# An attention and two-layer mixture kernel: one block's score and gate work reordered, and each expert's row numbers kept one expert earlier

## The reference, cut to what matters

```python
def _attn_ref(q, k, v):            # q, k, v: (2, 8, 576, 64)
    scores = scale * np.matmul(q, k.transpose(0, 1, 3, 2))
    kth = np.partition(scores, -top_k, axis=-1)[..., -top_k:-top_k + 1]     # top_k = 32
    scores = np.where(scores >= kth, scores, -1000000000.0)
    attn = np.exp(scores - np.max(scores, axis=-1, keepdims=True))
    attn = attn / (np.sum(attn, axis=-1, keepdims=True) + 1e-09)
    return np.matmul(attn, v)

def _moe_ref(x, w_in, w_out):      # x: (1152, 512), w_in: (512, 2048), w_out: (2048, 512)
    h = x @ w_in
    return (h * np.cos(h)) @ w_out

def _moe2_ref(x, w_gate, w1, w2, capacity):    # 8 experts, w1: (8, 512, 1024), w2: (8, 1024, 512)
    expert_idx = np.argmax(x @ w_gate, axis=1)
    # gate_w[i]: softmax weight of the chosen expert; each expert takes its first `capacity` rows
    h = np.maximum(np.einsum('ecd,edf->ecf', disp, w1), 0.0)
    y = np.einsum('ecf,efd->ecd', h, w2)
    out[i] = gate_w[i] * y[expert_idx[i], pos[i]]
```

## Time and profile before

| what | value |
|---|---|
| median of 3 runs | 662.5 us (661.8 to 662.95) |
| the profiled execution, its own time | 662.5 us |
| its span, first to last instruction | 660.8 us |
| TensorE matmul busy | 611.5 us, 93% |
| TensorE weight load busy | 548.3 us, 83% |
| VectorE busy | 526.6 us, 80% |
| ScalarE busy | 437.7 us, 66% |
| GpSimd busy | 289.7 us, 44% |
| chain that ended last | PE 66%, ACT 15%, POOL 8%, issue 7%, DVE 3% |

### The profile page before, as it was taken

One profiled execution on the slowest core, in us unless ns is written; L12 is line 12 of the kernel. 1 busy time (PEld: TensorE's weight loads), 2 busy tenths in 40 slices (PEclk: granted clock), 3 DMA queues, 4 the chain that ended last, 5 costly groups with the idle time before them and its releaser, 6 DMA issues.

```text
span 660.8 us, 13481 instructions
## 1 busy us (share of the span) xinstructions
PE 611.5 (93%) x4302; PEld 548.3 (83%) x4302; DVE 526.6 (80%) x1017; ACT 437.7 (66%) x727; POOL 289.7 (44%) x294
## 2 busy tenths in 40 slices
PE   4778798899999999999999999999898999999994
PEld 3556696798897898998988978989687999999994
DVE  5999999988989979989989985016539877789751
ACT  2567478679679679688596796736438665667630
POOL 0376559457477366566474675821500111011111
PEclk9988599999999999999999999999899999999998
DMA  5874700000000000000000000060398675675400
GB/s 180 354 325 172 270 5 5 26 5 5 25 5 5 25 6 5 25 9 1 28 4 16 0 0 18 1 235 5 144 348 303 231 269 199 248 248 221 147 18 16
DMA packets 17792, 68.62 MB, mean 104 GB/s; under 512 B 1998, under 2 KB 6606, under 8 KB 15056
## 3 DMA queue, kind: packets, MB, share of 16 engines
q1 hardware_dynamic: 16000, 63.27, 25.8%
q0 software_dynamic: 1744, 4.73, 2.0%
HBM read 54.33 MB, written 14.45 MB: 104 GB/s over the span
## 4 chain that ended last, share of the span: by engine, by line
PE 66%; ACT 15%; POOL 8%; issue 7%; DVE 3%; DMA 0%; POOLq 0%; ACTq 0%; SPq 0%; DVEq 0%
PE p_a L1281 8%; PE p_o L1243 6%; PE p_b L1281 5%; PE p_s L1205 5%; PE p_b L1303 4%; PE p_t L1222 3%; PE p_s L1498 3%; PE p_b L1305 3%; PE p_b L1304 3%; PE p_t L1498 3%; PE p_t L1475 3%; POOL arena L678 3%; PE p_s L1475 3%; ACT arena L843 2%; POOL w_out_lo L717 2%
## 5 line engine op out<-in xcount | busy, mean ns | idle before, releaser
L374 DVE MAX8 top<-arena 128x8 f32<-128x576 f32 x288 | 201.1, 745 | 7.4 <-ACT arena L843 7.3
L377 DVE MATCH_REPLACE8 arena<-top,arena 128x576 f32<-128x576 f32 x216 | 158.6, 741 | 0.0
L678 POOL TENSOR_TENSOR arena<-arena,pen 128x576 f32<-128x576 f32 x72 | 100.7, 1421 | 57.1 <-ACT pen L850 57.1
L1243 PEld LDWEIGHTS p_o<-arena,probsT 128*128 128x128 f32 (+1 forms) x720 | 85.7, 191 | 12.8 <-ACT probsT L870 6.8
L1243 PE MATMUL p_o<-arena,probsT 128*128 128x65 f32 (+1 forms) x720 | 90.9, 273 | 5.6 <-ACT probsT L870 3.8
L870 ACT COPY probsT<-p_t 128x384 f32<-128x384 f32 x108 | 51.3, 480 | 53.9 <-PE p_t L1222 53.8
L1222 PE MATMUL p_t<-ident,arena 128*128 128x128 f32 x324 | 55.7, 284 | 13.2 <-ACT arena L862 13.2
L1281 PE MATMUL p_a<-xT,wff 128*128 128x128 f32 x512 | 66.0, 283 | 0.0
L1281 PE MATMUL p_b<-xT,wff 128*128 128x128 f32 x512 | 64.3, 279 | 0.0
L1303 PE MATMUL p_b<-w_out_lo,g_hi 128*128 128x512 f32 x144 | 62.5, 434 | 1.9 <-ACT h_sb L889 1.6
L1281 PEld LDWEIGHTS p_a<-xT,wff 128*128 128x128 f32 x512 | 60.8, 195 | 2.8 <-issue 2.4
(11 more groups left out here) (186 smaller groups left out, 1309.4 us busy)
## 6 DMA issues: line engine op xcount, KB each, us to landing
arena<-in_w SPq DMA_DIRECT2D x8, 2048.0 KB, 9.0
wff<-in_w SPq DMA_DIRECT2D x8, 2048.0 KB, 9.1
slot_rows<-y_now SPq DMA_DIRECT2D x1, 4626.0 KB, 14.7
wff<-in_w_out SPq DMA_DIRECT2D x1, 4096.0 KB, 12.2
wff<-in_w_in SPq DMA_DIRECT2D x1, 4096.0 KB, 22.0
wff<-slot_rows SPq DMA_DIRECT2D x8, 385.5 KB, 3.7
arena<-in_vones SPq DMA_DIRECT2D x2, 1300.0 KB, 16.8
q_sb<-in_q SPq DMA_DIRECT2D x36, 64.0 KB, 1.9
```

The costliest lines, as they stand in the source:

```text
L374: nc.vector.max(best, src).then_inc(top_step, 1)
L377: nc.vector.match_replace(work[:, a, :], best, src, LOWEST).then_inc(top_step, 1)
L678: nc.gpsimd.tensor_tensor(s_sb[:, t, :], s_sb[:, t, :], pen[:, t % 2, :], ALU.subtract).then_inc(masked, 1)
L1243: last = mm(p_o[q, lo:lo + n], probsT[:, g % 2, P * c + q.start:P * c + q.stop], vones[b][:, p, at:at + n], start=(k == 0), stop=(k == PAI ...
```

## The change

Two things move; nothing is added or taken away.

In block 1, GpSimd makes the bias and the masks of pair 0 of block 2 ahead of the gate product of part 2, and ScalarE does the last score copy, the penalties and the exponentials of that pair ahead of the cosines of parts 2 and 3.

In the experts, VectorE's `keep` for expert E no longer stands inside expert E behind the scaling of expert E-1's rows. It stands inside expert E-1, behind `low_x(E)` and ahead of the rest of the weight splitting for expert E. With the indices of that place, its second wait is for the sending of expert E-2's rows, whose sending starts in the same expert E-1.

```diff
@@ VectorE, expert @@
                 else:
                     scale_rows(E - 1, 1 - j, turn - 1 + j, n)
-                    keep(E, j, turn, n)
                 sum_unit(E, 2, n)
...
                 if more:
                     low_x(E + 1, n)
+                    keep(E + 1, 1 - j, turn + j, n)
                     low_w1(E + 1, 1 - j, range(4) if begin else (2, 3))
                     low_w2(E + 1, 1 - j, 0)
                 sum_unit(E, 4, n)
@@ GpSimd, body, block 1 @@
                     fraction(i - 1, 3)
+                    bias(i + 1, 0)
+                    masks(i + 1, 0)
                     gated(i - 1, 2)
-                    bias(i + 1, 0)
                     gated(i - 1, 3)
-                    masks(i + 1, 0)
                     bias(i + 1, 1)
@@ ScalarE, second_body, block 1 @@
                 copy_pT(i, 10)
+                scores(i + 1, 3)
+                pens(i + 1, 0)
+                copy_pT(i, 11)
+                exps(i + 1, 0)
                 cosines(i - 1, 1)
-                scores(i + 1, 3)
-                copy_pT(i, 11)
-                pens(i + 1, 0)
+                copy_o(i, 1)
                 high_g(i - 1, 2)
-                copy_o(i, 1)
                 high_g(i - 1, 3)
-                exps(i + 1, 0)
                 pens(i + 1, 1)
```

## The result

| | before | changed |
|---|---|---|
| median | 662.7 us (4 runs, 661.8 to 664.5) | 687.1 us (4 runs, 684.8 to 689.6) |
| ratio | | 1.037, 95% interval 1.031 to 1.042 |
| profiled execution, own time | 662.5 us | 684.2 us |
| its span | 660.8 us | 682.4 us |

The change made the kernel 24 us slower. The four timed runs of the changed kernel fall into two pairs, at 684.9 and 689.5 us, with mean granted clocks of 0.970 and 0.973 in the one and 0.956 and 0.958 in the other; the profiled execution belongs with the faster pair.

What follows compares the result with a forecast made beforehand. The prediction took TensorE's pace to bound the experts and a wait for ScalarE to bound the end of block 1. It summed 662.5 + 3.1 - 0.1 + 15.7 = 681.2 us, range 671 to 691.

Steps and rivals of the forecast that it cites:

- The bound: Expert loop: TensorE sets the pace, busy 20.37 of 20.40 us; VectorE's 3.6 us to spare must cover `keep`'s cost.
- Block 1, exponentials: End of block 1: exponentials done at 113.2 and 114.65, TensorE's transposes at 115.1 without a wait, winning 2.4 us there.
- Block 1, what is late next: Cosines now behind exponentials: remainder at 119.4, w_out matmul at 119.5; the 2.4 us given back and 0.35 more.
- Blocks 2 and 3: Table load inside the loop: block 2's multiplication with v 2.1 us late, block 3 up to 1.0 more; 3.1 together.
- The drain of the table load: ScalarE in block 1's part: the skill page adds a 1.38 us drain per switch, making 5.9 us instead of 3.1.
- Five stalls, with expert 6 free for lack of a load: Experts 1 to 5: `keep` waits for a sending beside the w1 load; expert 0 has no wait, expert 6 no load.
- Size of a stall: Experts: last packet 4.2 us behind `low_x`, 0.3 until VectorE goes on, 0.15 of copies; weight splitting 4.4 us late.
- The alternative that I wrote down: Experts: if the rows' moving clears nothing, each stall is 5.4 us and costs 4.2, 21 us in all.
- Cover: Experts: the sum of unit 5 comes 1.24 us before `turn_back`'s second half needs it, hiding that much of each stall.
- The five stalls together: Five experts: 4.4 - 1.24 = 3.15 us for TensorE in each, 15.7 us.
- The copies, -0.1: `keep`'s two copies: 0.14 us won in each of experts 6 and 7, 0.14 lost in expert 0; sum -0.1 us.
- The clock: Rival: TensorE's clock falls behind six new pauses in experts and block 2, 688 us in all; chance 0.14.

Runs made afterwards that it cites:

- block 1 alone: Kernel before with only the block 1 reordering, `keep` at its old place: 665.3 us, ratio 1.004.
- the kernels with the later w1: SyncE starts the w1 load one unit of TensorE later, put on the kernel with only `keep` moved (662.3 us) and on the changed kernel (666.0 us).
- `keep` alone: Kernel before with only `keep` moved into the previous expert behind `low_x`, block 1 as before: 686.4 us, ratio 1.036.
- The changed kernel with the later w1: Changed kernel, with SyncE starting the w1 load of the expert after next one unit of TensorE later: 666.0 us, ratio 1.006.
- the late `keep`: Kernel before with `keep` moved one expert earlier, but to that expert's end, behind the last `low_w2`: 661.5 us, ratio 0.9987.
- the filled pauses: Kernel with only `keep` moved, plus three extra unread TensorE matmuls before `turn_back`'s first half in experts 1 to 6: 682.7 us, ratio 1.030.
- the later w1: Control: kernel before with only the w1 load started one unit of TensorE later, `keep` at its old place: 662.4 us, ratio 1.000.
- `keep` in between: Kernel before with `keep` moved one expert earlier, behind `low_w1` and the first `low_w2`, ahead of the sum of unit 4: 665.4 us, ratio 1.005.
- `keep` with the later w1: Kernel before with `keep` moved as in the changed kernel and the w1 load started one unit of TensorE later: 662.3 us, ratio 1.000.

## Why the prediction was right, and where it was off

- **The bound.** That the experts run at TensorE's pace and that VectorE's spare time decides: right. The stretch without a stall takes 20.43 us, the others 24 to 26.
- **Block 1, exponentials.** Forecast done at 113.2 and 114.65, transposes at 115.1 without a wait; measured 113.2 and 114.6, transposes at 114.61 without a wait. Right.
- **Block 1, what is late next.** The remainder was put at 119.4 and the w_out matmul at 119.5; it came at 119.78. Right in kind, 0.3 us low. The wait is 3.5 us and not the 2.9 that I named as its sign, because TensorE also got there 0.35 us earlier, at 116.26.
- **Blocks 2 and 3.** Load done and multiplication with v at 123.05, measured 123.08; the transposition of x at 125.4, measured 125.52; block 3 up to 1.0 more, measured 0.75. Sum forecast 3.1, measured 2.74 at the last block and 3.25 at the first expert, 2.9 us (1.7 to 4.0 by its interval) in the runs with this part alone. Right. In the profiled execution the clock was at half from 119.6 to 123.0 us; this cost nothing at the multiplication with v, since the copy that it needs came no sooner (block 1 alone, at full clock, waits 1.28 us for that copy). A kernel with the old block 1 also loses time here in some executions, 1.6 us as the last section shows, and the profiled one of before was not of them. That the single pair of traces gave so nearly the forecast is in part luck.
- **The drain of the table load.** The Trainium skill's 1.38 us (ScalarE: Activation LUTs, What ACT_TABLE_LOAD costs) would have made this part 5.9 us. The new loads took 1.28 us and the next instruction followed at once (121.19 and 122.48, 167.81 and 169.10); the trace does not bear the drain out.
- **Five stalls, with expert 6 free for lack of a load.** Right, and shown by the kernels with the later w1: the w1 load beside the sending is the cause.
- **Size of a stall: the term that came out too small.** VectorE idled 5.0 us instead of 4.5 and was 5.06 us late instead of 4.4. The forecast had three pieces. The last packet was put 4.2 us behind `low_x`, 5.2 less 0.9: "At the 430 GB/s or so of these loads this clears 0.9 us from the engines' way". This saving had no row of its own, and most of it came: 5.14 us before, 4.41 after, so 0.7 of the 0.9, and 0.2 us of the miss. The 0.3 us from the last packet until VectorE goes on were 0.60, with 1.18 in expert 2; this hand-over is the larger half, and no row stood behind it. The two copies hold VectorE for 0.25 us (530.07 to 530.32) and not 0.15. The alternative that I wrote down, nothing cleared and a cost of 4.2 us each, comes nearer to the 4.04, but not for its reason: its stall of 5.4 us is too long, and with the cover it gives 5.3 - 1.24 = 4.1.
- **Cover.** Right: 1.24 us forecast, 1.22 to 1.24 measured wherever the clock stayed up. 5.06 - 1.22 = 3.84 each, 19.2 us.
- **The five stalls together.** Forecast at 15.7 us, measured 20.2. Of the gap of 4.5 us the lateness of VectorE makes 3.3, the clock in experts 2 and 3 makes 1.1.
- **The copies, -0.1.** Nothing was won: the stretches that end with experts 6 and 7 take 20.43 and 18.73 us, as before. In expert 0 the copies cost 0.12 us where 0.14 were forecast.
- **The clock.** Given 0.14 as a case of its own. In the profiled execution it fell behind the pause in block 2 (0.50 from 120 to 123 us) and behind two of the five pauses in the experts, where it cost 1.1 us, for part of what TensorE lost in slow matmuls it saved in the next wait. In the trace of `keep` alone it fell behind all five and cost 3.2 us or more in these stretches. The two pairs of timed runs told of at the start differ in it. So it was not a rival to my case but lay on top of it, in some executions. The forecast ought to have carried half of it in the middle.
- **The sum.** In the trace 3.4 + 20.2 = 23.6 us; less 2.0 us for the last stretch it is the 21.6 of the spans. Against the 18.7 us forecast these 23.6 leave 4.9, of which the stalls make 4.5. In the medians 24.4 us: `keep` alone 24.0, block 1 alone 2.9, which add to 26.9, so together they are not worse than apart. The changed kernel with the later w1 takes 4.0 us more than before (2.6 to 5.6), in line with block 1's part.

## What to carry to other kernels

A wait that moves earlier in an in-order stream may be waiting for a different event, or for the same one much sooner; find out when that event comes in the trace of before, from the packets of the very DMA, and compare it with the moment at which the engine will arrive. Here a small scattered DMA issued together with a load of 2 MB landed more than 5 us later than without it: give such a wait a place behind the landing, or start the large load later; either made the 24 us vanish. The last packet is not yet the release: the engine went on 0.4 to 1.2 us behind it, and an estimate from packets must add that.

## What the runs showed of the hardware

**The clock behind a pause depends on the execution.** Seven of the twelve traces have block 1 as it was and TensorE's pause of 2.4 us in front of the same transposes. In four of them (the kernel before, the late `keep`, the filled pauses, the later w1) the granted clock stayed at 1.00 behind it; in three (`keep` alone, `keep` in between, `keep` with the later w1) it was 0.50 for 3.4 us. The transposition of x of block 2 came 14.5 us behind the cosines' table load in the four and 16.1 in the three, so a kernel with the old block 1 loses 1.6 us there in some executions. With block 1 changed, a pause of 3.2 us in front of the first w_out matmul was followed by full clock in one execution, and one of 3.3 us by 1.2 GHz for over 6 us in another. The Trainium skill (TensorE: Matmul & The Clock Gate, Part 1) says that the number of slow matmuls at a kernel's start varies from run to run of one kernel; here the same is seen of pauses in the middle. Doing 2.1 us of useless matmuls in pauses of 2.6 to 3.3 us kept the clock at 1.00 in the experts and was faster by 3.7 us.

**The end of the launch has two lengths.** From the last `turn_back` to the end of the span the executions took either 6.7 us (eight of the ten experiments' profiles, and the changed kernel) or 7.8 to 8.8 (the other two, and the kernel before). The last sending of before and of the changed kernel:

```profile
655.49 0.92 POOL L821 DMA_INDIRECT out_rows<-h_sb,own_number  x1 [0.31 <-issue]
...
679.08 0.91 POOL L820 DMA_INDIRECT out_rows<-h_sb,own_number  x1 [0.30 <-issue]
```

The first ends the span 5.3 us later, at 660.8, the second 3.3 us later, at 682.4, with the same instructions behind it. So two spans should be compared at a place before the end, here TensorE's last `turn_back`; 2 us of the kernel before were of this kind. Why it is so was not tried.

**A table load can land in a loop.** With the cosine's table left behind at the end of block 1, the load of the other one stood inside the loop's body and ran in each pass, in block 3 too, where nothing had changed the table since; that cost 1.1 us at the multiplication behind it and 0.8 us further on.
